# Two orders in a fused attention and expert kernel: when three experts' weights are sent for, and where the split weights stand in VectorE's prologue

## What is computed

```python
# 1 gated linear recurrence per head: B, H, S, D = 4, 8, 768, 48
mag = np.sqrt(a_re * a_re + a_im * a_im)
scale = np.minimum(mag, 0.999) / (mag + 1e-06)      # a_n = a * scale (complex)
for t in range(S):
    S_re, S_im = a_n[t] * S + k[t] v[t]^T           # complex state, D x D
    y[t] = q[t] @ S_re
# 2 dense MLP on x = y as (3072, 384): w_in 384 x 2048, w_out 2048 x 384
h = x @ w_in
x2 = (np.maximum(h, 0) + alpha * np.minimum(h, 0)) @ w_out
# 3 top-1 routed experts: E = 8, w1 384 x 1024, w2 1024 x 384
do_compute = x2 @ w_skip > 0                        # the others are passed through
e = argmax(x2 @ w_gate); gate = softmax(...)[e]
out = x2 + gate * (relu(x2 @ w1[e]) @ w2[e])
```

## Time and profile before

| | |
|---|---|
| device time, median of three runs | 968.17 us (966.34 to 971.03) |
| device time of the profiled execution | 968.83 us |
| span of the profiled execution | 966.9 us, mean granted TensorE clock 0.922 |
| prologue up to the first matmul of the recurrence | 0 to 82.1 us |
| phase 1, steady part | to 760 us |
| phase 2, up to the first matmul of an expert | 766.7 to 805.1 us |
| phase 2, experts | 805.1 to the end |
| TensorE busy, ScalarE busy, VectorE busy | 78%, 38%, 72% of the span |

### The profile page before, as it was taken

One profiled execution on the slowest core, in us unless ns is written; L12 is line 12 of the kernel. 1 busy time (PEld: TensorE's weight loads), 2 busy tenths in 40 slices (PEclk: granted clock), 3 DMA queues, 4 the chain that ended last, 5 costly groups with the idle time before them and its releaser, 6 DMA issues. The chain is left out here.

```text
span 966.9 us, 16131 instructions
## 1 busy us (share of the span) xinstructions
PE 751.7 (78%) x5478; PEld 723.3 (75%) x5479; DVE 699.2 (72%) x1231; ACT 367.4 (38%) x805; POOL 51.8 (5%) x48
## 2 busy tenths in 40 slices
PE   1343456987897989889798889979999547998786
PEld 1333456987886989788688788879999447998786
DVE  6967988988999799898899989875333373434333
ACT  5452234435434534433453353334433222322221
POOL 1000000000000000000000000000000012233122
PEclk9999567999999899999999999999999857999799
DMA  6542343243342424424242352233210393324520
GB/s 188 178 152 79 93 118 90 64 130 113 80 109 62 139 65 115 126 66 133 70 118 73 100 151 63 70 113 97 57 56 1 133 357 110 126 73 163 205 82 17
DMA packets 82433, 104.74 MB, mean 108 GB/s; under 512 B 15990, under 2 KB 68384, under 8 KB 82336
## 3 DMA queue, kind: packets, MB, share of 16 engines
q1 hardware_dynamic: 80544, 99.69, 35.2%
q0 software_dynamic: 1792, 3.76, 1.2%
HBM read 61.04 MB, written 12.19 MB: 76 GB/s over the span
## 5 line engine op out<-in xcount | busy, mean ns | idle before, releaser
L524 PE MATMUL out_ps<-w_out_hi,g_parts 128*128 128x394 f32 x768 | 225.3, 350 | 26.3 <-DVE g_parts L933 26.3
L514 PE MATMUL mlp_ps<-xT,w_in_hi 128*128 128x384 f32 x768 | 207.1, 351 | 20.3 <-DMA xT<-y_parts 8.6
L524 PEld LDWEIGHTS out_ps<-w_out_hi,g_parts 128*128 128x128 f32 x768 | 145.9, 193 | 30.3 <-DVE g_parts L933 30.2
L514 PEld LDWEIGHTS mlp_ps<-xT,w_in_hi 128*128 128x128 f32 x768 | 140.5, 194 | 27.5 <-issue 13.5
L928 DVE SCALAR_TENSOR_TENSOR g<-mlp_ps,slope_side,bent 128x384 f32<-128x384 f32 x128 | 78.6, 615 | 83.4 <-ACT bent L666 75.3
L524 PE MATMUL out_ps<-w_out_lo,g_parts 128*128 128x394 f32 x384 | 133.8, 348 | 0.0
L514 PE MATMUL mlp_ps<-xT,w_in_lo 128*128 128x384 f32 x384 | 131.2, 342 | 0.0
L666 ACT ACTIVATE bent<-mlp_ps,bend_size 128x384 f32<-128x384 f32 x128 | 73.7, 576 | 149.5 <-PE mlp_ps L514 149.0
L1303 PE MATMUL mlp_ps<-xT_e,w_sb 128*128 128x128 f32 x624 | 79.5, 290 | 19.3 <-issue 14.1
L1303 PEld LDWEIGHTS mlp_ps<-xT_e,w_sb 128*128 128x128 f32 x624 | 77.4, 205 | 22.1 <-issue 16.9
L672 ACT ACTIVATE g_parts<-g 128x384 fp32r<-128x384 f32 x128 | 66.2, 517 | 35.4 <-DVE g L928 35.4
(11 more groups left out here) (150 smaller groups left out, 1082.8 us busy)
## 6 DMA issues: line engine op xcount, KB each, us to landing
kq<-qk_dec SPq DMA_DIRECT2D x96, 144.0 KB, 3.0
w_sb<-in_w SPq DMA_DIRECT2D x8, 1536.0 KB, 7.7
w_raw<-in_w SPq DMA_DIRECT2D x8, 1536.0 KB, 12.0
gates<-in_a SPq DMA_DIRECT2D x24, 384.0 KB, 4.3
qk_raw<-in_qk SPq DMA_DIRECT2D x24, 384.0 KB, 4.2
xT<-y_parts SPq DMA_DIRECT2D x48, 144.0 KB, 2.8
v_nat<-in_v SPq DMA_DIRECT2D x24, 192.0 KB, 4.0
out<-x SPq DMA_DIRECT2D x8, 576.0 KB, 3.2
```

Source lines behind the costliest of these rows:

```text
L514: last = pe.matmul(ps[:, 0:HT], w_in_v[s][:, kk, f * P:(f + 1) * P], xT[n.p][:, kk, m, :], start=(kk == 0 and j == 0), stop=(kk == KT - 1 ...
L524: last = pe.matmul(out_ps[i][:, 0:DL], g_parts[:, f % 4, s, i * P:(i + 1) * P], w_out_v[m][:, f, :], start=(f == 0 and j == 0), stop=(f == ...
```

## The change

In phase 2, SP sends for expert 0 alone at the start, waits for the first gather (`x_gathered`) and then sends for experts 1, 2 and 3. In the prologue, VectorE's list takes two weight items behind each `scale_gates`, one behind each of the other steps, and items 20 and 21 between `sum_products` and `inverse`; ScalarE takes items 20 and 21 behind `square_products`.

```diff
@@ ScalarE, prologue
-            for kind, n in WEIGHT_ORDER:
-                if kind == "in":
-                    split_w_in(n)
-                else:
-                    split_pack(n)
+            def split_weights(first, last):
+                for kind, n in WEIGHT_ORDER[first:last]:
+                    if kind == "in":
+                        split_w_in(n)
+                    else:
+                        split_pack(n)
+
+            split_weights(0, 20)
             for c in range(NC):
                 square_products(Half(0, 0), c)
+            split_weights(20, 22)
             take_factors(Half(0, 0))
@@ VectorE, prologue
-            scale_gates(first_h, 0)
-            low_weights(0, 1)
-            scale_gates(first_h, 1)
-            low_weights(1, 2)
-            scale_gates(first_h, 2)
-            low_weights(2, 3)
+            for c in range(NC):
+                scale_gates(first_h, c)
+                low_weights(2 * c, 2 * c + 2)
             for j in range(1, SL):
                 within(first_h, j)
-                low_weights(2 + j, 3 + j)
+                low_weights(5 + j, 6 + j)
             for k in range(len(STEP_SHIFTS)):
                 across(first_h, k)
-                low_weights(10 + k, 11 + k)
+                low_weights(13 + k, 14 + k)
             for part in range(3):
                 carry_products(first_h, part)
-                low_weights(14 + 3 * part, 17 + 3 * part)
-            for c in range(NC):
-                sum_products(first_h, c)
+                low_weights(17 + part, 18 + part)
+            sum_products(first_h, 0)
+            low_weights(20, 21)
+            sum_products(first_h, 1)
+            sum_products(first_h, 2)
             inverse(first_h, 0)
             decay_qk(first_h, 0)
+            low_weights(21, 22)
             inverse(first_h, 1)
             inverse(first_h, 2)
@@ SP, phase 2
-            for p in range(BODY - 1):
-                load(0, p)
-            sp.wait_ge(table_full, 1)
-            load(0, BODY - 1)
+            load(0, 0)
+            sp.wait_ge(x_gathered, 16)
+            for p in range(1, BODY):
+                load(0, p)
```

## The result

The changed kernel takes 972.68 us (median of 19 runs, 967.88 to 978.52) against 968.17 us before (19 runs); the ratio is 1.0051, 95% interval 1.0034 to 1.0068. Two more comparisons, each against runs of the kernel before on the same chip, gave 1.0047 (1.0028 to 1.0066) and 1.0034 (1.0011 to 1.0057). So it is slower, by 3 to 5 us. The profiled execution of the changed kernel was the quickest of its nineteen: 967.88 us, span 966.0, against 968.83 and 966.9 before. Read by its span alone this profile would say "faster"; its parts have to be read one by one.

The account below looks back on a forecast made before the run. Bounds: phase 2's strict gather, copy, first product sequence, and VectorE's prologue waits, which phase 1 follows. Loads +9.8 less prologue 4.5 gave +5.3 us: 974.1 on the profile, 973.5 on the median, 973.8 said; 8-in-10 range 970.0 to 978.0.

Parts of the forecast that it names:

- The loads' half: Phase 2's start: gather takes 5.2 us, not 8.75, but ScalarE's copy waits for expert 1's w2 and begins 9.8 us later.
- the pair of loads: Phase 2: from first issue of expert 1's w1, w2 to ScalarE's split, taken as 11.6 us, bounds 10.99 and 12.30.
- the split's hold: Phase 2, ScalarE: split(0, 1) ahead of the copy, 2.76 us with a little overlapped, taken as 2.7 us.
- The prologue's half: VectorE's list: spread items wait less for packs, so q and k are decayed and scores follow 4.5 us earlier; bounds 2.5 to 7.8.
- The wait of 1.2 us forecast among the `across` steps: Prologue, VectorE: three packs among the short steps take about 5 us, so one wait of 1.2 us was expected there.
- The wait behind sum_products(0): Prologue, item 20: ScalarE makes its high part behind three squares, ready at 63.5, so VectorE idles for 2.5 us.
- One of the prediction's own tests: Phase 2: prediction wrong if the 161.8 us from first product (805.06) to span's end (966.9) changes by over 2 us.
- The prologue gives back more: VectorE's list, 49 to 69 us: prologue gains 7 us, copy is 9.2 late, total +2.2, 971.0; chance 0.26.
- The loads hinder more than the copy: 800 to 827 us: gathers and code fetches beside full queues cost +3 to +5 more, 977 to 979; chance 0.12.
- The prologue's gain does not reach the first chunk: Prologue: SP's factor moves, or ScalarE at item 20, take the gain; +9.8 us, 978.6; chance 0.06.
- The gather was not slowed by loads: Phase 2's first gather still takes 8.75 us, copy 13.3 late, +8.8, 977.6; chance 0.04.
- The rule of turns: DMA engine alternates queues packet by packet, so the gather loses about its own short length beside loads; basis of the 0.04 rival.

Follow-up runs that it names:

- three experts ahead: The whole change, but experts 0, 1 and 2 sent for at the start and only expert 3 behind the gather; 959.80 us, ratio to before 0.9938.
- two experts ahead of the gather: The whole change, but expert 1's loads ahead of the gather with expert 0's, experts 2 and 3 behind it; 959.02 us, ratio to before 0.9905.

## Why the prediction was right

**Direction and size.** +5.3 us were forecast, on the median 973.5, and 973.8 was said; 972.68 was measured, +4.5 by the medians, +0.51% by the ratio. That is inside the stated range of 970.0 to 978.0. The forecast stood near the edge between "same" and "slower", with 0.53 for slower, and the result lies on that edge: 0.51% in the first comparison, 0.47% and 0.34% in the other two, all three clear of zero. The two mechanisms were right, and the two terms were each somewhat too small, the loads' by about 0.5 us at the copy and the prologue's by about 0.6. That these misses offset each other in the sum is luck.

**The loads' half: +9.8 forecast.** The copy moved by 10.4 us in the first profile, and in all five profiles with this half it stood 20.0 to 20.2 us behind the gather's issue. Alone the half cost 8.3 and 9.7 us. The terms: the gather 5.2, measured 5.4 (5.3 to 5.4 in the nine profiles where the queues were empty, 8.8 to 9.0 in the other five); the pair of loads 11.6, measured 12.12 (794.05 to 806.17); the split's hold 2.7, measured 2.67. The small excess is mostly the pair's term. The prediction also worked out 9.2 us for the pair from the fit in the Trainium skill ("DMA: Bandwidth & Descriptors", Anatomy of one DMA) and left it unused. The page gives this fit for transfers issued by GpSimd, and these are issued by SP. A pair with no other load behind it took 10.84 us here, from 760.86 to the split at 771.70 in the changed kernel.

**The prologue's half: -4.5 forecast.** Masked scores on the mean of the profiles with the old prologue 85.9 (four), with the new one 81.2 (nine): 4.7 us. The change leaves the first piece of w_in at its place in every list, but this mean also holds when its load landed: ScalarE began on it between 14.6 and 16.4 us in the fourteen profiles, and what sets it is not shown. Counted from the start of that piece's low part to the start of the last products for q and k (16.15 to 72.63 before, 17.21 to 68.70 in the change), the prologue took 56.5 to 57.0 us in the four profiles and 51.4 to 51.8 in the nine: 5.2 us less, in each of them. So the term was too small. The wait of 1.2 us forecast among the `across` steps was not there; the 0.56 us stood behind them. VectorE's waits for packs fell to 2.8 us and not to about 4. The wait behind sum_products(0) was forecast at 2.5 us and was 2.19, but the high part that ended it came at 64.0 and not at 63.5: ScalarE's squares began at 60.41, when the last product had ended (60.37), and not half a microsecond before its end. By the start of phase 2 the gain was 5.1 us (766.1 and 761.0 on the mean of the same profiles), and the half alone timed at -7.1 and -6.2, with intervals whose upper ends are at 4.5 and 3.6 us. Whether there is more than the 5.1 or 5.2 us of the traces is not settled.

**The sum.** By the profiles: 5.1 us gained up to phase 2; 27.8 us from there to the gather's issue in every kernel; from the gather's issue to the end 171.1 us on the mean of the four profiles with the old loads and the same slots, 180.5 on the five with the new: 9.5 lost. Net +4.4, beside +4.9, +4.5 and +3.3 by the three ratios.

**One of the prediction's own tests failed.** It said it would be wrong if the stretch from first product to end changed by more than 2 us from 161.8. In the first profile it was 966.0 - 809.5 = 156.5, 5.3 us less. This is what made that execution the quickest. It is no step of the mechanism: the kernel before, profiled again, had 159.2 there, 2.6 us less than 161.8, and two further profiles of the changed kernel had 1.4 and 6.2 us more from the gather's issue to the end. At the ninth slot's copy the shift against before was still 10.7 us (103.7 and 93.0 us behind the gather's issue); the rest went at the turn to expert 4 and in the last slots. At that turn TensorE stood idle for 5.16 us in this execution and for 6.70 to 7.31 in the other thirteen profiles, which is 1.6 us of it. Later, and in other executions at other places, one first product or another of 48 matmuls takes 7.25 us and not 5.62 (in the repeated profile of the kernel before the one at 838.17, whose granted clock was 0.52 from 840 to 842). Which executions get the one or the other is not explained here. The test was too sharp for single profiles that differ by up to 6 us there.

**The rivals.** "The prologue gives back more" (0.26): by its own condition, a prologue's gain over 5 us, it came half true, with 5.1. What kept the sum from its 971.0 is the other half: it put the copy 9.2 us late, with a pair of 10.99, and the pair was longer and the copy 10.4 late. "The loads hinder more than the copy": later slots ran as before; the second gather, under full queues, took 6.6 us where it took 3.3, and was wanted much later. "The prologue's gain does not reach the first chunk": it does. "The gather was not slowed by loads": fell by five profiles with 8.8 to 9.0 us beside loads and nine with 5.3 to 5.4 without. The rule of turns in the Trainium skill ("DMA: Bandwidth & Descriptors", Queues, rings and completion order), as I had applied it, would have had the gather lose only its own short length; a gather beside full queues lost 3.3 to 3.7 us in these kernels. The rule itself may stand; that a small transfer is nearly unharmed does not follow from it. The same page's rule for authors, to issue early and wait late, agrees with what was measured on expert 1's load: sent for behind the gather it put the copy at 20.2 us, sent for ahead of it at 6.4. It does not hold for every load here: expert 3's went out early in the kernel before and cost the gather 3.4 us, and with three experts ahead, where it alone moved behind the gather, ScalarE's split of its w2 (at 824.23) still began without a wait.

## What to carry to other kernels

Before a transfer is moved behind another one to spare it contention, list every engine that waits for the moved transfer, and look at what stands behind that wait in the engine's own order: here 3.4 us of contention were saved and 14 us of waiting put on the path, because a copy stood third in a list behind a wait for the load. If only one of several loads is needed early, leave that one in front and move the rest: two experts ahead of the gather took the gain whole at the first slot and kept 2.3 us of it at the third, three experts ahead kept all 3.5 us. And in a list written by hand, an item costs the path its own work and all the time that it waits for another engine. Spread among the steps where its input was ready, an item did not wait; the last two, whose input was late, belonged behind the last instruction that the path needs, and in front of it the one at item 20 cost a wait of 2.19 us.

## What the hardware showed that was not expected

A product cut in two by an idle stretch of 9.67 us took 4.50 and 5.49 us for its halves of 24 matmuls, where the change's product of 48, in one piece, took 7.26: the level of the clock rose at the end of the first half, was lost in the idle stretch, and the second half ran at the lower level throughout. So starting TensorE early and letting it stop won 1.0 us at the second slot where the waits alone said 3.5.

Executions of one kernel differ by about 1% (967.88 to 978.52 us for the change), and the profiled one may be the quickest. A difference of half a per cent was visible in the ratio of nineteen runs and in the positions within the trace, but not in the span of one profile.
